# Batch 0 prepared by halves: what must stand before the first token tile, and what moves into it

## The chip, the cores and the metric

The kernel runs on one core of a Trainium2 chip. The core has TensorE (PE), VectorE (DVE), ScalarE (ACT), GpSimd (POOL) and SyncE (SP); each runs its own instructions in order, and they wait for each other by semaphores. The metric is the device time of one execution in microseconds.

## The reference

Two attentions with softmax, then two feed-forward blocks, all in float32. B = 8 batches, H = 8 heads, 576 tokens of 64 dimensions a head, 32 packed queries `p`:

```
p_packed = softmax(p @ k^T / 8) @ v          # 32 x 64 a head
attn     = softmax(q @ p_packed^T / 8) @ p_packed
x        = attn as 4608 tokens x 512
xn       = x / sqrt(mean(x * x) + 1e-6) * rms_g
y        = (silu(xn @ w_gate) * (xn @ w_val)) @ w_out     # 512 -> 1536 -> 512
h        = y @ w_in                                        # 512 -> 2048
out      = (max(h, 0) + alpha * min(h, 0)) @ w_out2        # 2048 -> 512
```

## The kernel before

The first block runs over 16 token tiles of 288 tokens: `tile(b, half, at)`, two halves for each of 8 batches. The second block runs over 9 tiles of 512 tokens and is not touched. A product in the tiles is three matmuls: every operand is split into a rounded `hi` part and a rest `lo` (`three_passes`, L476 to L478: hi x hi, lo x hi, hi x lo).

The value projection of the second attention is folded into the weights: for each batch `folded` (L606) multiplies the packed values by `w_gate` and `w_val`; the result m (12 blocks of 256 columns for two groups of heads) is split into `m_hi` and `m_lo`. Six folds, `fold0` to `fold5`, give two blocks each. A tile then multiplies the normed probabilities `an_hi`, `an_lo` by m.

Before tile 0 batch 0 is prepared on all engines (I call it the preparation). In order: scores of `p` against the keys in two halves (L497), copy to SBUF (L759), maximum, exp, sum, division (L919 to L934), transposes (L510), packed values (L523), their transpose, token scores for both halves (L548), transposes back (L951), softmax over 32 keys in each half (`shift`, `probs`, `sums`, `turn_p`), attention output `x` (L575) only for its squares (L795), two sums on POOL (L418, L420), a mean by a matmul with a constant (L584), `rsqrt` as exp of -0.5 ln (L803, L805) and one Newton step on DVE, `normed` on POOL (L424), and the split into `an_hi` (ACT, L811) and `an_lo` (DVE, L1006). The first preparation is `beside(0, name)` for a list of names on each of PE, ACT and DVE; those lists are the order in their queues. POOL's order is written out below `const_in`; after batch 0's steps it splits the twelve `w_out` chunks (`ow_hi` L436, `ow_lo` L438). Batch c = 1 to 7 is prepared inside the two tiles of batch c - 1: `PE_PLACES`, `DVE_PLACES` and `ACT_PLACES` name the work for each place of a tile, as `(half, where, step)`.

A tile has 12 steps f: products of gate and value (12 matmuls), Silu on ACT, the product `act_sb` on DVE (L1052), `h_hi` (ACT, L859) and `h_lo` (DVE, L1055); two steps later 12 matmuls with `w_out` accumulate the output. In PE's stream the places are "within" (between gate and value), "after", and "between" (after the output's matmuls).

Before some steps of the preparation PE runs fillers (`keep_busy`, L691): fp32 matmuls of a constant, whose result nobody reads, two instructions each; six of them stand last before tile 0. All loads go through SP's queue in the order of the code: p, k in two pieces, v, q, two small tables, four pieces of w_gate and w_val (`gv`), then a wait for the token scores, two pieces of w_out (`ow`), and batch 1's p and k.

## Time and profile before

| | |
|---|---|
| median of 3 timed runs | 1590.81 us (1589.01 to 1592.89) |
| the profiled execution | 1593.56 us, its span 1591.8 us |
| PE busy | 1566.0 us, 98% of the span |
| DVE, ACT, POOL busy | 727.9, 487.7, 206.2 us |
| mean granted PE clock | 0.992 |
| DMA | 76.18 MB, 48 GB/s over the span |

### The profile page before, as it was taken

Reading aid. Unit: us, or ns where it says so; the run is one execution under the profiler, and the core shown is the slowest. Engines: PE = TensorE matmul, PEld = TensorE weight load, DVE = VectorE, ACT = ScalarE, POOL = GpSimd, SP = SyncE. Lnnn points to the kernel's source line nnn. Section 1 sums busy time; section 2 is a strip of 40 time slices with the busy share of each in tenths; the row PEclk is TensorE's granted clock in tenths of the full one; section 3 lists DMA queues with packets and bytes.
Section 4 is the critical chain, followed back from the end, with each engine's and each line's share of the span. In section 5 each row is a group of like instructions: output and inputs, shape, how many; then the busy total and the mean of one; then the engine's idle time right before and its main releaser. Section 6 shows DMA issues by size and latency. Waiting matters only on the chain.

```text
span 1591.8 us, 25845 instructions
## 1 busy us (share of the span) xinstructions
PE 1566.0 (98%) x10390; PEld 1319.4 (83%) x10390; DVE 727.9 (46%) x1264; ACT 487.7 (31%) x913; POOL 206.2 (13%) x148
## 2 busy tenths in 40 slices
PE   6999999999999999999999999999999999999998
PEld 2688979888898888979988888888888888888887
DVE  4555454554545555454453334344434434343343
ACT  3445445463545545443211111111111111111111
POOL 1701010010100001013670101010100101010000
PEclk8899999999999999999999999999999999999999
DMA  9111202121030211103130101010000001010000
GB/s 356 66 46 47 73 5 77 45 77 46 2 107 16 77 46 46 44 3 148 42 121 0 54 0 53 0 40 13 26 26 26 26 0 53 0 53 0 23 4 27
DMA packets 38627, 76.18 MB, mean 48 GB/s; under 512 B 2192, under 2 KB 11408, under 8 KB 38544
## 3 DMA queue, kind: packets, MB, share of 16 engines
q1 hardware_dynamic: 33360, 65.55, 11.9%
q10 hardware_dynamic: 5184, 9.44, 1.5%
q8 instruction: 62, 1.02, 0.3%
q14 instruction: 21, 0.17, 0.0%
HBM read 56.11 MB, written 18.87 MB: 47 GB/s over the span
## 4 chain that ended last, share of the span: by engine, by line
PE 94%; DVE 3%; ACT 1%; issue 1%; POOL 0%; ACTq 0%; DVEq 0%; POOLq 0%
PE psum L476 30%; PE psum L477 28%; PE psum L478 28%; PE psum L606 2%; PE psum L575 1%; PE psum L691 1%; PE psum L497 1%; DVE m_lo L1012 1%; PE psum L523 1%; PE psum L548 1%; PE psum L584 1%; PE psum L510 1%; DVE h_lo L1055 1%; DVE act_sb L1052 0%; ACT h_hi L859 0%
## 5 line engine op out<-in xcount | busy, mean ns | idle before, releaser
L1088 DVE TENSOR_TENSOR h_lo<-g,h_hi 128x512 fp32r<-128x512 f32 x144 | 124.5, 865 | 453.0 <-ACT h_hi L886 453.0
L886 ACT CAST h_hi<-g 128x512 fp32r<-128x512 f32 x144 | 89.4, 621 | 637.3 <-PE psum L478 570.7
L476 PE MATMUL psum<-an_hi,m_hi 128*128 128x288 f32 x768 | 236.7, 308 | 3.7 <-DVE act_sb L1052 3.7
L476 PE MATMUL psum<-h_hi,ow_hi 128*128 128x288 f32 x768 | 235.9, 307 | 0.0
L477 PE MATMUL psum<-h_hi,ow_lo 128*128 128x288 f32 x768 | 227.2, 296 | 0.0
L477 PE MATMUL psum<-an_hi,m_lo 128*128 128x288 f32 x768 | 226.7, 295 | 0.0
L478 PE MATMUL psum<-h_lo,ow_hi 128*128 128x288 f32 x768 | 225.8, 294 | 0.0
L478 PE MATMUL psum<-an_lo,m_hi 128*128 128x288 f32 x768 | 225.7, 294 | 0.0
L1052 DVE TENSOR_TENSOR act_sb<-act_sb,psum 128x288 f32<-128x288 f32 x192 | 86.9, 453 | 190.2 <-PE psum L478 181.7
L476 PEld LDWEIGHTS psum<-an_hi,m_hi 128*128 128x128 f32 x768 | 144.0, 187 | 36.0 <-issue 28.5
L476 PEld LDWEIGHTS psum<-h_hi,ow_hi 128*128 128x128 f32 x768 | 144.1, 188 | 34.8 <-issue 33.5
L1055 DVE TENSOR_TENSOR h_lo<-act_sb,h_hi 128x288 fp32r<-128x288 f32 x192 | 104.7, 546 | 101.7 <-ACT h_hi L859 101.2
L477 PEld LDWEIGHTS psum<-h_hi,ow_lo 128*128 128x128 f32 x768 | 144.6, 188 | 0.4
L477 PEld LDWEIGHTS psum<-an_hi,m_lo 128*128 128x128 f32 x768 | 144.4, 188 | 0.6 <-issue 0.2
L478 PEld LDWEIGHTS psum<-h_lo,ow_hi 128*128 128x128 f32 x768 | 144.5, 188 | 0.0
L478 PEld LDWEIGHTS psum<-an_lo,m_hi 128*128 128x128 f32 x768 | 144.3, 188 | 0.0
L476 PE MATMUL psum<-xs,w_hi_front 128*128 (+1 forms) x360 | 140.1, 389 | 0.5 <-ACT y_sb L869 0.5
L476 PE MATMUL psum<-h_hi,w_hi_front 128*128 128x512 f32 x360 | 140.6, 391 | 0.0
L478 PE MATMUL psum<-h_lo,w_hi_front 128*128 128x512 f32 x360 | 140.1, 389 | 0.0
L477 PE MATMUL psum<-h_hi,w_lo_front 128*128 128x512 f32 x360 | 140.1, 389 | 0.0
L477 PE MATMUL psum<-xs,w_lo_front 128*128 (+1 forms) x360 | 140.0, 389 | 0.0
L478 PE MATMUL psum<-xs,w_hi_front 128*128 (+1 forms) x360 | 140.0, 389 | 0.0
(124 smaller groups left out, 2427.2 us busy)
## 6 DMA issues: line engine op xcount, KB each, us to landing
k_sb<-k_t SPq DMA_DIRECT2D x16, 576.0 KB, 4.6
q_sb<-q_t SPq DMA_DIRECT2D x8, 1152.0 KB, 6.4
y_mid<-y_sb SPq DMA_DIRECT2D x16, 576.0 KB, 3.4
xs_raw<-y_mid SPq DMA_DIRECT2D x9, 1024.0 KB, 5.2
out_t<-o_sb ACTq DMA_DIRECT2D x36, 256.0 KB, 2.0
v_sb<-v_s SPq DMA_DIRECT2D x8, 1024.0 KB, 6.5
gv_sb<-w_gv SPq DMA_DIRECT2D x4, 1536.0 KB, 18.2
w_raw_front<-w SPq DMA_DIRECT2D x2, 2560.0 KB, 13.0
```

The costliest lines, as they stand in the source:

```text
L476: nc.tensor.matmul(dst, w_hi, hi, start=start, stop=False)
L477: nc.tensor.matmul(dst, w_lo, hi, start=False, stop=False)
L478: return nc.tensor.matmul(dst, w_hi, lo, start=False, stop=stop)
L497: mm = nc.tensor.matmul(scores_ps[PACK * pair:PACK * (pair + 1), e, :], p_sb[dims, pair, :], k_sb[dims, pair, h * HALF:(h + 1) * HALF], st ...
L510: mm = nc.tensor.transpose(at_ps[t][:, at:at + P], a_sb[:, g, KEY_STARTS[j]:KEY_STARTS[j] + P], ident[:])
L523: mm = nc.tensor.matmul(pp_ps[PACK * pair:PACK * (pair + 1), e * HEAD_DIM:(e + 1) * HEAD_DIM], a_t[:, j, col:col + PACK], v_sb[:, j, head ...
L548: mm = nc.tensor.matmul(s2_ps(e)[PACK * pair:PACK * (pair + 1), :], pp_t[dims, pair, :], q[dims, pair, h * HALF:(h + 1) * HALF], start=Tru ...
L606: mm = nc.tensor.matmul(psum[keys, m_bank(c, j) + e, :].rearrange("p (f n) -> p f n", f=2), pp_tg[dims, pair, :], gv_sb[dims, 2 * j:2 * j ...
L886: nc.scalar.copy(h2_hi[:, f % 2, :], g32[:, f % 2, :]).then_inc(g_hi_done, 1)
L1052: nc.vector.tensor_tensor(act_sb[:, s, :], act_sb[:, s, :], val_ps, ALU.mult).then_inc(h32_done, 1)
L1055: nc.vector.tensor_tensor(h_lo[:, s, :], act_sb[:, s, :], h_hi[:, s, :].bitcast(F32), ALU.subtract).then_inc(h_lo_done, 1)
L1088: nc.vector.tensor_tensor(h2_lo[:, s, :], g32[:, s, :], h2_hi[:, s, :].bitcast(F32), ALU.subtract).then_inc(g_lo_done, 1)
```

## The change

Batch 0's preparation before tile 0 keeps half 0's chain, and the six folds. Half 1's `sums`, `probs`, `turn_p`, x2, x3, mean, rsqrt, Newton, norm and split get places in tile 0 (`PE_FIRST`, `DVE_FIRST`, `ACT_FIRST`), with the second halves of fold2 on DVE and of fold5's copy on ACT. Folds 3 to 5 are copied whole by ACT into `m_raw`, and POOL splits them (`split_m`), between the chunks of `w_out`. For batch 0 scores stay in PSUM (the maximum and exp read them there), the two POOL sums become a mean of four accumulating matmuls, half 0 is normed by DVE (`normed0`), half 1's `shift` subtraction is POOL's. k is loaded by halves of keys, `ow` in three pieces without a wait. Six fillers before the tile go, others come between. The diff, cut to what the prediction speaks of:

```diff
-FILLERS = {"scores0": 3, "scores1": 1, "turn_a01": 2, "packed": 1, "turn_packed": 1, "tokens0": 1, "tile": 6}
+PE_FIRST = {
+    (0, "after", 3): ["x2"], (0, "between", 3): ["x3"], (0, "between", 4): ["mean1"],
+}
+DVE_FIRST = {
+    (0, "within", 0): ["fold2"], (0, "after", 1): ["sums1"], (0, "between", 1): ["probs1"], (0, "after", 2): ["turn_p1"],
+    (0, "within", 5): ["mean1"], (0, "between", 7): ["newton1", "normed1"], (0, "within", 10): ["split1"],
+}
+ACT_FIRST = {
+    (0, "after", 0): ["fold5"], (0, "after", 3): ["x2"], (0, "between", 3): ["x3"],
+    (0, "between", 6): ["rsqrt1"], (0, "within", 9): ["split1"],
+}
+EARLY_BANK, LATE_BANK = 7, 0
+FILLERS = {"scores0": (3, EARLY_BANK), "scores1": (1, EARLY_BANK), "turn_a01": (4, EARLY_BANK),
+           "packed": (1, LATE_BANK), "turn_packed": (1, LATE_BANK), "tokens0": (1, LATE_BANK),
+           "x0": (2, LATE_BANK), "fold2": (1, LATE_BANK), "fold3": (1, LATE_BANK), "fold5": (1, LATE_BANK)}
+SPLIT_BY_POOL = 3
...
+        m_raw = place("m_raw", [P, NF1, GROUPS, GV], F32, at=m_lo_at)
...
-        q0_sb = place("q0_sb", [P, PAIRS, SEQ], at=ow_at)
+        q0_at = ow_at + 4 * 3 * MODEL
+        q0_sb = place("q0_sb", [P, PAIRS, SEQ], at=q0_at)
+        rinv_0 = place("rinv_0", [P, 2, HALF], at=q0_at + 4 * PAIRS * SEQ)
+        mean_0 = place("mean_0", [P, 2, HALF], at=q0_at + 4 * PAIRS * SEQ + 2 * step)
+        e2_0 = place("e2_0", [P, 2, GROUPS, HALF], at=q0_at + 4 * PAIRS * SEQ + 4 * step)
...
+        sq_0 = place("sq_0", [P, PAIRS, HALF], at=y_at)
...
+            return 0 if first(c) and i == 0 else 2
         def m_bank(c, j):
...
-            return 4 + 2 * (j % 2) if first(c) else 2
+            return [4, 6, 4, 6, 2, 6][j] if first(c) else 2
+
...
                 def at(where, f):
+                    if c == 1:
+                        for name in starting.get((half, where, f), []):
+                            beside(0, name)
...
-                for g in range(GROUPS):
-                    pairs = slice(2 * g, 2 * g + 2)
-                    sp.dma_start(k_sb[:, pairs, :],
-                                 k_t[b].rearrange("(c p) s -> p c s", p=P)[:, pairs, :]).then_inc(k_in[g], 16)
+                for h in range(2):
+                    keys = slice(h * HALF, (h + 1) * HALF)
+                    sp.dma_start(k_sb[:, :, keys],
+                                 k_t[b].rearrange("(c p) s -> p c s", p=P)[:, :, keys]).then_inc(k_in[h], 16)
...
-            sp.dma_start(g_sb[:], rms_g).then_inc(const_in, 16)
-            sp.dma_start(alpha_sb[:], alpha).then_inc(const_in, 16)
+            sp.dma_start(g_sb[:], rms_g).then_inc(g_in, 16)
...
-            sp.wait_ge(s2_mm, 2)
-            for n in range(2):
-                chunks = slice(n * NF1 // 2, (n + 1) * NF1 // 2)
+            for n in range(3):
+                chunks = slice(n * NF1 // 3, (n + 1) * NF1 // 3)
                 sp.dma_start(ow_raw[:, chunks, :], w1_o[chunks].rearrange("f p n -> p f n")).then_inc(ow_in[n], 16)
+            sp.dma_start(alpha_sb[:], alpha).then_inc(alpha_in, 16)
+            sp.wait_ge(scores_mm, 2)
...
+            def shift1():
+
+                pool.wait_ge(sub2_done, 1)
+                pool.wait_ge(s2_turned, 4)
+                pool.wait_ge(max2_done, 2)
+                rows = e2_0[:, 1].rearrange("p g s -> p (g s)").rearrange("p (b k) -> p b k", k=PACK)
+                nc.gpsimd.tensor_tensor(rows, rows, max2[:, 1, :].unsqueeze(2).to_broadcast([P, GROUPS * BLOCKS, PACK]),
+                                        ALU.subtract).then_inc(sub2_done, 1)
+
+            def split_m(j):
+
+                n = j - SPLIT_BY_POOL
+                blocks = slice(2 * j, 2 * j + 2)
+                pool.wait_ge(m_raw_done, n + 1)
+                nc.gpsimd.tensor_copy(m_hi[:, blocks], m_raw[:, blocks]).then_inc(m_part, 1)
+                pool.wait_ge(m_part, n + 1)
+                nc.gpsimd.tensor_tensor(m_lo[:, blocks], m_raw[:, blocks], m_hi[:, blocks].bitcast(F32),
+                                        ALU.subtract).then_inc(m_split, 1)
+
+            pool.wait_ge(g_in, 16)
             scaled(0)
-            squares(0, 0)
-            normed(0, 0)
-            squares(0, 1)
-            normed(0, 1)
+            shift1()
+            split_m(3)
             for f in range(NF1):
-
-                pool.wait_ge(ow_in[f // (NF1 // 2)], 16)
+                if f == 3:
+                    split_m(4)
+                    pool.wait_ge(s2_mm, 2)
+                if f == 5:
+                    split_m(5)
+                if f == 7:
+                    pool.wait_ge(a2n_done, 2)
+                pool.wait_ge(ow_in[f // (NF1 // 3)], 16)
                 nc.gpsimd.tensor_copy(ow_hi[:, f, :], ow_raw[:, f, :]).then_inc(ow_hi_done, 1)
                 pool.wait_ge(ow_hi_done, f + 1)
                 nc.gpsimd.tensor_tensor(ow_lo[:, f, :], ow_raw[:, f, :], ow_hi[:, f, :].bitcast(F32),
...
+                pe.wait_ge(k_in[h], 16 * (c + 1))
                 if h == 0:
-                    for g in range(GROUPS):
-                        pe.wait_ge(k_in[g], 16 * (c + 1))
                     pe.wait_ge(p_in, 16 * (c + 1))
-
-                    reached(pe, mean_copied, 2 * c)
-                    reached(pe, m_lo_done, NF1 * c)
-                else:
-                    pe.wait_ge(scores_out, 2 * c + 1)
+                    if c == 1:
+
+                        pe.wait_ge(m_raw_done, 2)
+                    elif c > 1:
+                        pe.wait_ge(mean_copied, 2 * c)
...
-                        mm = nc.tensor.matmul(scores_ps[PACK * pair:PACK * (pair + 1), e, :], p_sb[dims, pair, :],
+                        dst = psum[PACK * pair:PACK * (pair + 1), 2 * e + h if first(c) else 2 + e, 0:HALF]
...
-                nc.tensor.matmul(mean_ps, mean_w[:], sq[:, 0, :], start=True, stop=True).then_inc(mean_mm, 1)
+                if first(c):
+                    for pair in range(PAIRS):
+                        pe.wait_ge(squared, 1 + pair // 2 if h == 0 else 4)
+                        mm = nc.tensor.matmul(mean_ps(c, h), mean_w[:], sq_0[:, pair, :], start=pair == 0,
+                                              stop=pair == PAIRS - 1)
+                    mm.then_inc(mean_mm, 1)
...
                 if first(c):
                     pe.wait_ge(gv_in[(2 * j + 1) * W1_GROUPS // NF1], 16)
-                    reached(pe, m_lo_done, 2 * (j - 1))
+                    if j in (2, 3):
+                        pe.wait_ge(m_lo_done, 2 * (j - 1))
+                    if j == 4:
+                        pe.wait_ge(squared, 2)
+                    if j == 5:
+                        pe.wait_ge(m_raw_done, 1)
...
-                        if half == 0:
-                            pe.wait_ge(m_lo_done, NF1 * b + 2 * (f // 2) + 2)
+                        if half == 0 and b == 0 and f // 2 >= SPLIT_BY_POOL:
+                            pe.wait_ge(m_split, f // 2 - SPLIT_BY_POOL + 1)
+                        elif half == 0:
...
+                        if n == 0 and d == 0:
+                            pe.wait_ge(m_lo_done, 2 * SPLIT_BY_POOL)
+                            pe.wait_ge(m_raw_done, SPLIT_BY_POOL)
...
-            def keep_busy(count):
+            def keep_busy(count, bank):
                 for _ in range(count):
-                    nc.tensor.matmul(psum[:, 1, :].rearrange("p (a n) -> p a n", n=P), mean_w[:],
+                    nc.tensor.matmul(psum[:, bank, :].rearrange("p (a n) -> p a n", n=P), mean_w[:],
                                      ident[:].unsqueeze(1).to_broadcast([P, BANK // P, P]), start=True, stop=True)
-            pe.wait_ge(consts_set, 4)
-            for name in ("scores0", "scores1", "turn_a01", "turn_a2", "packed", "turn_packed", "tokens0", "tokens1"):
-                keep_busy(FILLERS.get(name, 0))
-                if name in ("scores0", "scores1", "tokens0", "tokens1"):
+            pe.wait_ge(consts_set, 2)
+            for name in ("scores0", "scores1", "turn_a01", "turn_a2", "packed", "turn_packed", "tokens0", "fold0", "tokens1",
+                         "fold1", "x0", "x1", "mean0", "fold2", "fold3", "fold4", "fold5"):
+                if name in FILLERS:
+                    keep_busy(*FILLERS[name])
+                if name in ("scores0", "scores1", "tokens0", "tokens1") or name[:4] == "fold":
                     beside(0, name + "_ready")
                 beside(0, name)
-            for name in ("fold0", "fold1", "fold2", "x0", "x1", "fold3", "mean0", "x2", "x3", "fold4", "fold5", "mean1"):
-                if name[:4] == "fold":
-                    beside(0, name + "_ready")
-                beside(0, name)
-            keep_busy(FILLERS["tile"])
             tiles_of_a(pe, tile, beside)
...
                 act.wait_ge(m_mm, NF1 // 2 * c + j + 1)
+                if first(c) and j >= SPLIT_BY_POOL:
+                    bank = m_bank(c, j)
+                    nc.scalar.copy(m_raw[:, 2 * j:2 * j + 2].rearrange("p f e n -> p e f n"),
+                                   psum[:, bank:bank + 2, :].rearrange("p e (f n) -> p e f n", f=2)).then_inc(m_raw_done, 1)
+                    return
...
-            for name in ("scores0", "scores1", "exp0", "exp1", "turn_a0", "turn_a2", "packed", "probs0", "fold0", "probs1",
-                         "fold1", "fold2", "x0", "x1", "fold3", "rsqrt0", "x2", "x3", "split0", "fold4", "fold5", "rsqrt1"):
+            for name in ("exp0", "exp1", "turn_a0", "turn_a2", "packed", "probs0", "fold0", "fold1", "x0", "x1", "probs1",
+                         "rsqrt0", "fold2", "fold3", "silu", "split0", "fold4"):
...
-                dve.wait_ge(scores_out, 2 * c + 2)
-                nc.vector.tensor_reduce(negmax[:, g:g + 1], a_sb[:, g, :], AXIS.X, ALU.max,
-                                        negate=True).then_inc(max1_done, 1)
+                if first(c):
+                    dve.wait_ge(scores_mm, 2)
+                    nc.vector.tensor_reduce(negmax[:, g:g + 1], scores0_of(g), AXIS.XY, ALU.max,
+                                            negate=True).then_inc(max1_done, 1)
...
+            def normed0(h):
+                dve.wait_ge(newton_step, 3 * h + 3)
+                nc.vector.tensor_tensor(a2[:, h], a2[:, h], rinv_0[:, h, :].unsqueeze(1).to_broadcast([P, GROUPS, HALF]),
+                                        ALU.mult).then_inc(a2n_done, 1)
...
-            def folded(c, j):
-                for e in range(2):
-                    dve.wait_ge(m_hi_done, NF1 * c + 2 * j + e + 1)
+            def folded(c, j, parts=(0, 1)):
...
             for name in ("max0", "max1", "norm0", "norm1", "turn_a1", "packed", "turn_s0", "shift0", "turn_s1", "sums0",
-                         "probs0", "turn_p0", "shift1", "fold0", "sums1", "probs1", "turn_p1", "fold1", "fold2",
-                         "fold3", "mean0", "newton0", "split0", "fold4", "fold5", "mean1", "newton1"):
+                         "probs0", "turn_p0", "shift1", "fold0", "fold1e0", "mean0", "fold1e1", "newton0", "normed0",
+                         "split0"):
```

## Rows read from the trace of the kernel before

**Rows 1.** The page: busy time by engine (share of the span), instructions.
```profile
PE 1566.0 (98%) x10390; PEld 1319.4 (83%) x10390; DVE 727.9 (46%) x1264; ACT 487.7 (31%) x913; POOL 206.2 (13%) x148
```

**Rows 2.** Windows by stage: length, then busy time (instructions) of PE, PEld, DVE, ACT, POOL; clock, DMA share, GB/s.
```profile
7.36:24.86 17.50, 13.45 (x200) 5.57 (x199) 7.58 (x19) 5.09 (x11) 0.40 (x1) 1.00 1.04 380
24.86:27.84 2.98, 0.01 (x2) 0.00 (x0) 2.84 (x6) 0.78 (x2) 0.00 (x0) 1.00 1.03 412
27.84:46.69 18.85, 12.95 (x101) 3.46 (x101) 13.52 (x24) 12.00 (x20) 6.17 (x5) 0.50 0.86 316
46.69:51.73 5.04, 5.04 (x7) 2.03 (x6) 2.31 (x5) 2.31 (x4) 1.53 (x2) 0.50 0.00 0
```

**Rows 3.** Timeline of PE, 0 to 56 us: start, length, engine, line, what, count.
```profile
2.47 5.26 PE L691 MATMUL psum<-ident,mean_w 128*128 128x512 f32 x6 [2.47 <-POOL v_sb L397]
...
7.90 0.72 PE L497 MATMUL psum<-k_sb,p_sb 64*32 64x288 f32 x16 [0.17 <-issue]
...
10.26 1.98 PE L691 MATMUL psum<-ident,mean_w 128*128 128x512 f32 x4
...
16.20 0.44 PE L510 MATMUL psum<-ident,a_sb 128*128 128x128 f32 x2 [0.24 <-ACT a_t L773]
...
22.94 1.93 PE L606 MATMUL psum<-gv_sb,pp_tg 64*32 64x512 f32 x32
...
46.69 7.83 PE L691 MATMUL psum<-ident,mean_w 128*128 128x512 f32 x12
53.96 0.69 PE L476 MATMUL psum<-an_hi,m_hi 128*128 128x288 f32 x1
```

**Rows 4.** Timeline of DVE, 0 to 75 us.
```profile
11.18 0.75 DVE L919 TENSOR_REDUCE negmax<-a_sb 128x1 f32<-128x576 f32 x1 [11.18 <-ACT a_sb L759]
...
26.80 0.78 DVE L983 STREAM_TRANSPOSE a<-e 128x576 f32<-128x576 f32 x1
...
38.51 0.46 DVE L989 TENSOR_SCALAR mean_sb<-psum 128x288 f32<-128x288 f32 x1 [0.26 <-PE psum L584]
...
43.61 1.25 DVE L1006 TENSOR_TENSOR an_lo<-a,an_hi 128x576 fp32r<-128x576 f32 x1 [2.22 <-ACT an_hi L811]
...
57.88 0.46 DVE L1052 TENSOR_TENSOR act_sb<-act_sb,psum 128x288 f32<-128x288 f32 x1 [0.23 <-PE psum L478]
...
64.11 0.75 DVE L1006 TENSOR_TENSOR an_lo<-a,an_hi 128x576 fp32r<-128x576 f32 x1
...
71.39 1.29 DVE L1055 TENSOR_TENSOR h_lo<-act_sb,h_hi 128x288 fp32r<-128x288 f32 x1 [0.50 <-ACT h_hi L859]
```

**Rows 5.** Timeline of ACT, 33 to 44 us.
```profile
33.54 1.19 ACT L795 ACTIVATE sq<-psum 128x576 f32<-128x576 f32 x2
...
37.44 1.28 ACT L800 ACT_TABLE_LOAD   x1
...
42.91 0.67 ACT L811 CAST an_hi<-a 128x576 fp32r<-128x576 f32 x1 [1.92 <-POOL a L424]
```

**Rows 6.** Timeline of POOL, 36 to 75 us.
```profile
36.30 0.79 POOL L420 TENSOR_TENSOR sq<-sq 128x288 f32<-128x288 f32 x1
41.47 1.41 POOL L424 TENSOR_TENSOR a<-a,rinv 128x576 f32<-128x576 f32 x1 [4.38 <-DVE rinv L1001]
...
71.07 1.29 POOL L438 TENSOR_TENSOR ow_lo<-ow_raw,ow_hi 128x512 fp32r<-128x512 f32 x1
...
73.22 1.29 POOL L438 TENSOR_TENSOR ow_lo<-ow_raw,ow_hi 128x512 fp32r<-128x512 f32 x1
```

**Rows 7.** Timeline of PE's weight loads, 20.7 to 25 us.
```profile
23.67 0.29 PEld L606 LDWEIGHTS psum<-gv_sb,pp_tg 64*32 64x32 f32 x16 [0.57 <-DMA gv_sb<-w_gv]
```

**Rows 8.** Timeline of PE in tile 0 and the next, 70 to 126 us.
```profile
70.94 0.40 PE L476 MATMUL psum<-an_hi,m_hi 128*128 128x288 f32 x1 [0.91 <-DVE act_sb L1052]
...
117.21 0.71 PE L575 MATMUL psum<-a,pp 32*64 32x288 f32 x8
...
125.55 0.65 PE L584 MATMUL psum<-sq,mean_w 128*128 128x288 f32 x2
```

More of the change, by code:

```diff
@@ L212, in first, with e2_of, sq_of, mean_of @@
             return isinstance(c, int) and c == 0
+        def e2_of(c):
+            return e2_0 if first(c) else e2
+        def sq_of(c):
+            return sq_0 if first(c) else sq
+        def mean_of(c):
+            return mean_0 if first(c) else mean_sb
+        def rinv_of(c):
+            return rinv_0 if first(c) else rinv
+        def at_ps(c, t):
+            if t == 2:
+                return psum[:, 4 if first(c) else 2, 0:GROUPS * P]
+            return psum[:, 2 + t, :]
+        def mean_ps(c, h):
+            return psum[:, 1 if first(c) and h == 0 else 3, 0:HALF]
         def x_bank(c, i):
-            return 2 * (i % 2) if first(c) else 2
+            return 0 if first(c) and i == 0 else 2
         def m_bank(c, j):
-            return 4 + 2 * (j % 2) if first(c) else 2
+            return [4, 6, 4, 6, 2, 6][j] if first(c) else 2
+        def scores0_of(g):
+            return psum[:, 2 * g:2 * g + 2, 0:HALF]
+        def evicted(c):
+            return NF1 * c - 2 * SPLIT_BY_POOL if c else 0
         def y_ps(m):
@@ L579, in mean @@
             def mean(c, h):
-                if not first(c):
-                    pe.wait_ge(m_lo_done, NF1 * c + 6 + 4 * h)
-                pe.wait_ge(sq_part, 4 * c + 2 * h + 2)
-                nc.tensor.matmul(mean_ps, mean_w[:], sq[:, 0, :], start=True, stop=True).then_inc(mean_mm, 1)
+                if first(c):
[4 more added lines that the diff above has]
+                    mm.then_inc(mean_mm, 1)
+                else:
+                    pe.wait_ge(m_lo_done, evicted(c) + 6 + 4 * h)
+                    pe.wait_ge(sq_part, 4 * (c - 1) + 2 * h + 2)
+                    nc.tensor.matmul(mean_ps(c, h), mean_w[:], sq[:, 0, :], start=True, stop=True).then_inc(mean_mm, 1)
             def fold_ready(c, j):
@@ L763, in scores_exp @@
                 act.wait_ge(bias1_done, GROUPS * c + g + 1)
-                nc.scalar.activation(a_sb[:, g, :], a_sb[:, g, :], ACT.Exp, bias=bias1[:, g:g + 1],
-                                     scale=SCALE, accum_out=sum1[:, g:g + 1]).then_inc(exp1_done, 1)
+                nc.scalar.activation(halves(a_sb[:, g, :]), scores0_of(g) if first(c) else halves(a_sb[:, g, :]), ACT.Exp,
+                                     bias=bias1[:, g:g + 1], scale=SCALE,
+                                     accum_out=sum1[:, g:g + 1]).then_inc(exp1_done, 1)
             def turn_a(c, t):
-                if t == 0:
-                    reached(act, mean_mm, 2 * c)
+                if t == 0 and c > 1:
+                    act.wait_ge(mean_mm, 2 * c)
                 act.wait_ge(at_mm, 3 * c + t + 1)
@@ L772, in turn_a @@
                 dst = a_t[rows, 2 * t:min(2 * t + 2, CHUNKS), :]
-                nc.scalar.copy(dst.rearrange("p j n -> p (j n)"), at_ps[t][rows, :]).then_inc(at_act, 1)
+                nc.scalar.copy(dst.rearrange("p j n -> p (j n)"), at_ps(c, t)[rows, :]).then_inc(at_act, 1)
             def packed(c):
@@ L860, in tile @@
                     at("between", f)
-                    if half == 0 and f == 1:
+                    if half == 0 and f == 1 and b > 0:
                         split(b, 1)
@@ L1057, in tile @@
                     at("between", f)
-                    if half == 0 and f == 2:
+                    if half == 0 and f == 2 and b > 0:
                         split(b, 1)
```

109 lines of the change are left out of this document (66 added, 43 removed).

## Prediction, made before the changed kernel was run

> **What bounds the kernel now.** I read the page's list of engines first: PE is busy for 98% of the span [rows 1], so after the start the time is PE's own work, and only two things can move it: when the first token tile begins, and what PE does or waits for once it has begun. Then the windows by stage [rows 2]: up to 24.86 us PE runs mostly at full clock, then it stands still for 3 us and the granted clock goes to 0.50 (1.2 GHz of 2.4), where it stays through the rest of the preparation. The PE timeline [rows 3] shows how that ends: six fillers (12 instructions) from 46.69 us, in which the clock returns at 51.73, and the first matmul of the tile at 53.96. The DVE, ACT and POOL timelines [rows 4 to 6] give the chain in front of it: scores, softmax over keys, packed values, token scores, softmax, mean of squares, rsqrt and Newton, `normed`, `split0`. Of that only half 0 and `fold0` to `fold2` are needed by the first products; half 1 and folds 3 to 5 stand in the same queues.
>
> **The change, part by part.** I follow the new order of each engine with the durations of the rows; all times are from the start of the span.
>
> *Up to the keys' softmax.* PE now waits for two constants, not four: fillers start about 0.9 us earlier (1.55 instead of 2.47) and their six instructions of 5.26 us at 1.2 GHz end at 6.8 [rows 3]. `scores0` needs only the first half of the keys; the last k load of before was what `scores0` waited for at 7.90 (PE idle 0.17 there). `scores0` ends at about 8.0, one filler (1.98 for two, so 0.99) at 9.0, `scores1` at 9.7. The maximum is read straight from PSUM, so the copy is gone: it starts at 9.8 instead of 11.18 [rows 4], 1.35 earlier. Four fillers (4.0 us) end at 13.7, level with the normed scores. The last transposes no longer wait for ACT's copy (0.24 [rows 3]), so all that follows to the end of `turn_p0` is 1.6 earlier: 26.80 + 0.78 becomes 26.0 [rows 4]. Reading PSUM instead of SBUF could cost 0.1 or save 0.1 an operation; I take nothing.
>
> *Loads.* Splitting k by keys halves the pieces. I take 0.3 us later for all that lands behind it, bounds 0 and 0.6. The weight load for `fold1` lands when PEld waited for it, at 23.67 [rows 7], so about 23.9 now; two more gv loads of 1536 KB follow at about 400 GB/s [rows 2], so the last lands at 31.6, ahead of fold4. The ow loads are issued right behind and no longer wait for the token scores; the DMA engines are full until past 40 us either way (share 1.03, then 0.86 of 18.85 us, which is to 44 [rows 2]), so they land as before.
>
> *PE from there.* tokens0, fold0 (0.97, half of the 1.93 for two [rows 3]), tokens1 are done at 21.6; PE stands 2.3 us for gv; fold1 23.9 to 24.9; two fillers to 26.8; x0 and x1, about 0.5 each, to 27.8. Each Square is 0.6 [rows 5]. `mean0` is now four matmuls on PE instead of two POOL sums (1.41 + 0.79 [rows 6]) and one matmul: 4 x 0.56 (0.65 for one with its tail at full clock [rows 8]), done at 30.2. Bounds 1.9 and 2.6. Then filler, fold2, filler, fold3: 3.9, ending at 34.0.
>
> *Half 0's chain.* `mean_sb` starts at 30.3; before, `normed` started 2.96 after it (38.51 to 41.47 [rows 4, 6]); now it runs on DVE, in 0.76 instead of POOL's 1.41, done at 34.0. But `split0` has fold3's raw copy and a table load ahead of it on ACT: the copy, 1024 elements a partition, I put at 1.05 by the Square of 576 (0.6), bounds 0.9 and 1.3. So 34.1, copy to 35.15, table load 1.28 [rows 5] to 36.45, cast 0.67 to 37.15. The table load is put ahead of the tile so that Silu finds it loaded; it costs the chain 1.28.
>
> *The subtraction that ends it.* `an_lo` takes 0.75 on DVE when undisturbed, but 1.25 beside a POOL operation at 43.61 [rows 4]. In the tile an `h_lo` that starts at 71.39 ends at 72.68, 0.32 after the POOL subtraction of 71.07 + 1.29 [rows 4, 6]: the DVE operation with two SBUF inputs is held until POOL's is done. Now `split_m(3)` starts on POOL at 35.2, at the same moment as ACT's table load, and its operations are 1024 wide: cast about 1.2, subtraction 1.41 + 448 x 0.62/288 (the slope from 0.79 for 288 to 1.41 for 576 [rows 6]) = 2.4, that is from 36.4 to 38.8. `an_lo`, ready at 37.2, then ends at 39.1, not 37.95. The first tile matmul comes at 39.2, when fold4, filler and fold5 (34.0 to 36.9) are long done. That is 14.8 us before 53.96.
>
> The Trainium skill ("SBUF — State Buffer", section "Who interferes with whom") calls the shared port an exclusive lock for the whole instruction, for DVE operations with two SBUF inputs against POOL operations that read SBUF. The sum by the longest extra in the rows (0.83, on `h_lo`) would put the tile at 38.8; by the rule, with wider POOL operations, it is the 39.2 used. The rows at 71 us agree with the rule.
>
> *What the tile gets.* On PE: x2, x3 (0.71 each with tail [rows 8], 0.5 in a row) and `mean1` (2.3): 3.3 us added, all of it on the path, since PE is the bound. On ACT and DVE: fold2's halves, fold5's copy, two Squares, a table load pair, `sums1`, `probs1`, `turn_p1`, Newton, `normed1`. ACT and DVE have time in a step of 3.2 us, but in step 2 `probs1` and an `h_lo` stand in DVE's queue ahead of the product that PE's step 3 needs; before, the product of step 1 ended 4.4 after the tile's first matmul (57.88 + 0.46 [rows 4]), now at 43.6; `sums1` 1.3, `h_lo` 0.46, `probs1` 0.76 and the product 0.46 bring it to 46.6, and PE asks at about 48.2. So undisturbed it is 1.6 in time; behind one cast and subtraction of `split_m(4)` (3.6, less 0.5 that they overlap) it is 1.5 late. I take 0.7, between the two. The stall of 0.91 at step 5 [rows 8] goes: `mean1` fills PE there. Key loads for batch 1 fall due at 43 us, when they land; I take nothing, bound 0.5. POOL's 12 units of cast and subtraction repeat every 2.15 (71.07 to 73.22 [rows 6]); with three double ones among them they end near 73 at that price, and unit n is always 2 us or more ahead of PE. Unit 7 waits for `normed1`; by my order it is ready about 1.7 before PE's step 9 asks.
>
> *Sum.* 14.8 earlier, minus 3.3, minus 0.7, plus 0.9: 11.7 us. The profiled execution took 1593.56 us (span 1591.8, 1.8 around it), so it becomes 1581.9; it lay 2.75 above the median of the timed runs, 1590.81, so I predict 1579.1. Everything behind tile 0 has the same instructions and keeps its time.
>
> **Rivals.** (1) *The clock falls in the preparation.* For it: in the rows it fell after PE had stood idle for 3 us behind light work [rows 2]; the new order has a 2.3 us gap for gv between small matmuls, and another just ahead of the tile. Against it: in 7.36 to 24.86 it stayed up with PE busy 13.45 of 17.5 and gaps in it. Price: fold1, two fillers, x and mean0 at half speed put 5 us on the chain (a filler is 1.75 instead of 0.99, a mean of 0.56 double that), and the folds some more unless the clock returns first: 5.5 in all, 1584.6. The Trainium skill ("TensorE: Matmul & The Clock Gate", section "HAM oscillation — how this bites in real kernels") says that waits between groups of matmuls bring the gate back down; that speaks for this rival, and the trace's fall at 27.84 agrees.
> (2) *Nothing is held by POOL.* If the operations miss each other, the tile starts at 38.0 and step 3 does not stall: 1.2 + 0.7 more, 1577.2.
> (3) *DVE's queue in tile 0 becomes the bound.* If the 1.5 of step 3 comes back in each of the eight steps up to the last one with added work, 11 us are given back: 1590, no change. Against it: the heavy steps are few.
> (4) *POOL becomes the bound, slower than before.* It has 18 units (three double ones count two each) between 35.2 and PE's last step of tile 0 near 81. At 2.15 they end at 74. Above 2.55 a unit PE starts to wait; above 3.2 the wait exceeds the 11.7 gained. With DVE's new two-input operations in the same steps holding POOL in turn, 3.6 a unit gives 18 x 3.6 + 35 = 100, 19 late: 1598. The longest pair in the rows is far from that.
>
> **Chances.** Forecast 0.60 (its own range 1576 to 1582), rival 1 0.19, rival 2 0.12, rival 3 0.05, rival 4 0.04. The range 1575.0 to 1585.0 holds the first three with their costs' bounds (mean 0.4, loads 0.3, copy 0.3, stall 0.7) and leaves out the last two. A measurement of this kernel tells about 0.2%, 3.2 us, from no change. Faster by more than that 0.91, within 0.05, slower 0.04.
>
> **What would show it.** In the profile after: scores' maximum near 9.8 us; PEld waiting for gv near 23.9; `mean_sb` at 30.3 and no POOL sum before it; an `an_lo` longer than 1 us that ends right behind a POOL subtraction of 2.4 us; first tile matmul at 39.2 with the granted clock at 1.00 throughout from 8 us on; one idle of PE around 48 us behind `act_sb`; nothing different from tile 1 on. A clock of 0.50 anywhere between 24 and 45 us means rival 1; idle of PE behind `ow_lo` or `m_lo` of POOL means rival 4; a first tile matmul later than 45 us makes the prediction wrong.

## The result, and the profile after

The kernel after took 1587.70 us, median of 12 runs (1586.31 to 1588.86), beside 1590.70 for the kernel before on the same chip (12 runs, 1588.82 to 1593.05): a ratio of 0.9982 (0.9973 to 0.9990). It is faster by 3.0 us, not by 11.7, and lies above the range of 1575 to 1585. Its profiled execution took 1586.99 us (span 1585.2), 6.6 less than the profiled one of before.

The page's list of engines, after, answers to [rows 1]: PE has almost the same work in a shorter span.

```profile
PE 1566.3 (99%) x10404; PEld 1321.6 (83%) x10404; DVE 734.6 (46%) x1259; ACT 487.4 (31%) x909; POOL 211.5 (13%) x149
```

The windows by stage of the kernel after (columns as in [rows 2]):

```profile
7.03:23.02 15.99, 13.61 (x188) 5.91 (x186) 7.90 (x19) 4.05 (x10) 0.40 (x1) 1.00 1.04 385
23.02:25.03 2.01, 2.01 (x17) 0.68 (x18) 1.87 (x5) 1.25 (x3) 0.00 (x0) 0.72 1.03 410
25.03:27.30 2.27, 2.27 (x4) 0.67 (x2) 2.27 (x5) 0.30 (x1) 1.06 (x1) 0.50 1.02 410
27.30:40.57 13.27, 10.14 (x95) 3.50 (x94) 5.93 (x9) 8.88 (x12) 4.15 (x4) 1.00 1.06 376
40.57:44.37 3.80, 3.80 (x17) 3.80 (x18) 1.60 (x3) 1.58 (x3) 3.64 (x5) 0.55 0.83 278
```

The reader is to see two falls of the granted clock to 0.50 (1.2 GHz): one in the preparation, one as the tile begins. Both come within 1 us after PE had stood idle for 2 us or more, which its timeline after shows (start, length, what, count, idle before; answers to [rows 3]):

```profile
23.02 1.18 PE L704 MATMUL psum<-gv_sb,pp_tg 64*32 64x512 f32 x16 [2.01 <-DMA gv_sb<-w_gv]
24.13 3.54 PE L794 MATMUL psum<-ident,mean_w 128*128 128x512 f32 x4
27.61 0.74 PE L662 MATMUL psum<-a,pp 32*64 32x288 f32 x16
29.09 2.21 PE L671 MATMUL psum<-sq,mean_w 128*128 128x288 f32 x8 [0.74 <-ACT sq L896]
...
40.57 0.40 PE L556 MATMUL psum<-an_hi,m_hi 128*128 128x288 f32 x1 [2.39 <-DVE an_lo L1126]
...
42.34 0.44 PE L558 MATMUL psum<-an_lo,m_hi 128*128 128x288 f32 x1
42.58 0.44 PE L556 MATMUL psum<-an_hi,m_hi 128*128 128x288 f32 x1
```

After 2.01 us without work (for gv, as in [rows 7]) two fillers take 3.54 where two took 1.98 [rows 3]. After 2.39 us for `an_lo`, the tile's matmuls come every 0.24 us. At 46 us they come every 0.13.

DVE after, 38 to 52 us (answers to [rows 4]), then ACT, 35 to 38 us, and POOL, 36 to 50 us (answer to [rows 5, 6]):

```profile
38.39 2.13 DVE L1126 TENSOR_TENSOR an_lo<-a,an_hi 128x576 fp32r<-128x576 f32 x1 [3.37 <-ACT an_hi L912]
...
47.50 2.53 DVE L1177 TENSOR_TENSOR h_lo<-act_sb,h_hi 128x288 fp32r<-128x288 f32 x1
49.95 1.16 DVE L1092 TENSOR_TENSOR e<-e,rcp 128x576 f32<-128x576 f32 x1
51.04 0.44 DVE L1174 TENSOR_TENSOR act_sb<-act_sb,psum 128x288 f32<-128x288 f32 x1
```

```profile
35.36 1.01 ACT L918 COPY m_raw<-psum 128x1024 f32<-128x1024 f32 x1 [1.00 <-PE psum L704]
36.39 1.28 ACT L949 ACT_TABLE_LOAD   x1
37.68 0.67 ACT L912 CAST an_hi<-a 128x576 fp32r<-128x576 f32 x1
```

```profile
36.43 1.04 POOL L498 CAST m_hi<-m_raw 128x1024 fp32r<-128x1024 f32 x1 [9.04 <-ACT m_raw L918]
37.55 2.35 POOL L500 TENSOR_TENSOR m_lo<-m_raw,m_hi 128x1024 fp32r<-128x1024 f32 x1
...
47.33 2.38 POOL L500 TENSOR_TENSOR m_lo<-m_raw,m_hi 128x1024 fp32r<-128x1024 f32 x1
```

`an_lo` (0.75 undisturbed) stands beside POOL's subtraction and takes 2.13. At 47.50 `h_lo`, 288 wide, takes 2.53 beside the next one; the product behind it is late at 51.04. PE's waits from 40 to 94 us, after (line, for what, us in total, times, longest), where [rows 8] had one of 0.91:

```profile
PE psum L556 <- DVE an_lo L1126: 2.4, 1, 2.4
PE psum L556 <- DVE h_lo L1177: 1.0, 1, 1.0
PE psum L594 <- DVE mean L1103: 0.4, 1, 0.4
PE psum L556 <- DVE act_sb L1174: 0.3, 1, 0.3
PE psum L556 <- DVE e L1063: 0.2, 1, 0.2
```

The product that is late at 51.04 is the 0.3 for `act_sb`. The 1.0 for `h_lo` is another one, in the tile's last step. These rows of POOL, DVE, ACT and PE are its chain: POOL takes up its last `w_out` chunks only at 76.22, behind `normed1`; beside one of them DVE's subtraction for batch 1 takes 1.40 (0.76 undisturbed, last fence); ACT's exp waits for it, and the cast `h_hi` stands behind the exp.

```profile
76.22 0.61 POOL L516 CAST ow_hi<-ow_raw 128x512 fp32r<-128x512 f32 x1 [13.93 <-DVE a L1121]
...
85.99 1.30 POOL L518 TENSOR_TENSOR ow_lo<-ow_raw,ow_hi 128x512 fp32r<-128x512 f32 x1
```

```profile
86.50 1.40 DVE L1078 TENSOR_TENSOR e<-e,max 128x576 f32<-128x576 f32 x1
```

```profile
87.99 1.28 ACT L884 ACT_TABLE_LOAD   x1 [1.09 <-DVE e L1078]
...
90.35 0.41 ACT L965 CAST h_hi<-act_sb 128x288 fp32r<-128x288 f32 x1
```

```profile
91.40 0.37 PE L556 MATMUL psum<-h_hi,ow_hi 128*128 128x288 f32 x1 [0.96 <-DVE h_lo L1177]
```

Before, with POOL idle from 84 to 99 us, the same subtraction of DVE:

```profile
93.53 0.76 DVE L964 TENSOR_TENSOR e<-e,max 128x576 f32<-128x576 f32 x1
```

I measure tile 0 from its first matmul to the issue of the store of its result, 0.69 us on the SP queue: before from 53.96 to 100.98, after from 40.57 to 93.83.

So the tile starts 13.4 earlier and takes 53.3 instead of 47.0.

### The profile page after: what moved, and what is told of

Same layout as the page of the kernel before. It is cut to its first block, busy times and chain, and to the rows that moved or that the text cites. A ratio compares the mean times of both kernels' runs of the same rounds, so it can differ in the third digit from the quotient of the medians.

```text
span 1585.2 us, 25879 instructions
## 1 busy us (share of the span) xinstructions
PE 1566.3 (99%) x10404; PEld 1321.6 (83%) x10404; DVE 734.6 (46%) x1259; ACT 487.4 (31%) x909; POOL 211.5 (13%) x149
## 4 chain that ended last, share of the span: by engine, by line
PE 92%; DVE 4%; ACT 1%; issue 1%; DMA 1%; SPq 0%; ACTq 0%; DVEq 0%
PE psum L556 29%; PE psum L557 28%; PE psum L558 28%; PE psum L704 2%; PE psum L662 1%; DMA gv_sb<-w_gv 1%; DVE h_lo L1177 1%; DVE act_sb L1174 1%; ACT h_hi L965 1%; DVE m_lo L1132 1%; PE psum L594 0%; PE psum L580 0%; PE psum L634 0%; PE psum L609 0%; PE psum L677 0%
## 5 line engine op out<-in xcount | busy, mean ns | idle before, releaser
L1210 DVE TENSOR_TENSOR h_lo<-g,h_hi 128x512 fp32r<-128x512 f32 x144 | 129.0, 896 | 448.6 <-ACT h_hi L992 448.6
```

The costliest lines, as they stand in the source:

```text
L1210: nc.vector.tensor_tensor(h2_lo[:, s, :], g32[:, s, :], h2_hi[:, s, :].bitcast(F32), ALU.subtract).then_inc(g_lo_done, 1)
```

## The experiments

Three questions came out of this. Is the kernel before's profiled execution a fair base? What do the two falls of the clock cost? What does POOL's subtraction cost? Every kernel has its ratio to before with its 95% interval. Each difference that is smaller than an interval is called so. The twelve kernels ran in three groups of four, and the kernel before, measured beside each, had medians of 1591.24, 1590.50 and 1591.31 us (1590.70 beside the kernel after). A difference of medians across groups is uncertain by up to 0.8 us more; the ratios are not.

**The kernel before, again.** No edit.

> The kernel before, unchanged, to see its runs one by one with span and mean granted clock. The profiles put the changed kernel 6.6 us ahead (1593.56 to 1586.99), the medians 3.0. Theory phase: the profiled run of before was a slow sample; its time scatters by 4 us because the stretch at 1.2 GHz in the preparation begins and ends at another point in each run. Then the slower runs have the lower mean clock, and in a new profile the first tile matmul (53.96 before) moves by 2 us or more with the length of the slow stretch (23.9 us before). Theory rest: the clock is the same in all runs and the 3.6 us come from elsewhere (after tile 0, or outside the span); then the first tile matmul stays within 0.5 us of 53.96 in a profile of any time.

Measured: 1590.77 us (1589.28 to 1593.37), ratio 0.9997 (0.9989 to 1.0006); the profiled execution took 1590.77. The windows of its preparation (clock third from the end):

```profile
14.00:17.70 3.70, 3.06 (x11) 2.39 (x12) 1.24 (x3) 0.95 (x2) 0.00 (x0) 0.54 1.03 407
27.88:34.71 6.83, 3.15 (x32) 0.58 (x32) 6.66 (x12) 3.08 (x6) 0.00 (x0) 0.50 1.04 389
38.12:44.95 6.83, 6.41 (x50) 1.47 (x50) 2.56 (x6) 3.87 (x8) 2.78 (x2) 0.50 0.83 297
```

Here the clock fell three times and came back in between; in [rows 2] it stayed at 0.50 from 27.84 to 51.73. The tile starts at 51.58, not 53.96. The same program falls at other moments in other executions, and its time follows: mean granted clock 0.995 goes with 1588.5 to 1589.3, 0.994 with 1588.8 to 1590.9, 0.993 with 1591.0 to 1592.8, 0.992 with 1592.8 to 1593.5. The prediction's base, 0.992 and 1593.56, was at the slow end of that.

**The kernel before without its six fillers.** `"tile": 6` becomes `"tile": 0`.

> The kernel before without the six fillers ahead of tile 0 (7.8 us of PE in its profile, 46.69 to 54.5). Theory clock: their place is taken by the tile's first products at 1.2 GHz, so little is won: the tile starts at about 47 instead of 52 to 54, runs its first 3.4 to 6.8 us at half speed (1.7 to 3.4 us lost), 1 to 3.5 us off the time. Rival: the fillers are pure cost, 5 to 7 us off, and then most of what the changed kernel gains (3.0) could be had by taking them out.

Measured: 1588.53 us (11 runs), ratio 0.9985 (0.9976 to 0.9994). Tile 0 starts at 45.17, 6.4 earlier than in the run above, and at full clock (1.00 from 45.17 to 50.50). But ACT is busy with half 1's rsqrt and then with Silu's table load until 49.09, and PE waits for the first Silu:

```profile
49.66 0.37 PE L476 MATMUL psum<-an_hi,m_hi 128*128 128x288 f32 x1 [2.53 <-ACT act_sb L853]
```

After that wait the granted clock is 0.51 from 50.50 to 54.00. The store is issued at 96.28 instead of 98.03. Leaving out the six alone gives 2.0 us; by the ratios this kernel and the kernel after (0.9982) are not told apart.

**The old order, with fillers to keep its clock up.** The six are left out and these come in:

```diff
+                if name == "fold2":
+                    keep_busy(5)
+                if name == "mean0":
+                    pe.wait_ge(squared, 1)
+                    keep_busy(1)
+                if name == "mean1":
+                    pe.wait_ge(squared, 3)
+                    keep_busy(2)
```

> The kernel before with its order kept, but fillers where PE stands idle (five ahead of fold2, one ahead of mean0, two ahead of mean1) and none of the six ahead of the tile. Nothing moves into tile 0. Theory clock: the preparation stays at 2.4 GHz, the chain to mean1 loses about 3 us and the tile starts at 43 to 44 at full speed, with none of the 3 us of x2, x3 and mean1 in the tile: 7 to 9 us off the time of before, more than the change's 3.0. Rival order: what counts is that half 1's chain stood ahead of the tile; then the clock alone gives under 3 us.

Measured: 1588.90 us (12 runs), ratio 0.9993 (0.9985 to 1.0002), tile from 46.52, where 7 to 9 us were expected. The fillers were too few in places: the clock still fell three times, for 10 us in all, the last time as the tile began. No gain over the run before. So whether the old order at full clock would reach the new one isn't shown; all that follows builds on the new order.

**Two fillers in the gap ahead of fold1.**

```diff
-           "x0": (2, LATE_BANK),
+           "fold1": (2, LATE_BANK), "x0": (2, LATE_BANK),
```

> The changed kernel with two fillers ahead of fold1, where PE stood 2.0 us for the gv load and the clock fell at 23.94 for 3.4 us. Theory clock: the clock stays up, x0 comes 0.8 earlier, mean 0.8 to 1.0 earlier, and the tile 0.8 to 1.3 earlier; the runs scatter less. Rival: fold1 is only moved by the fillers, which end at 23.0 + 0.3, nothing gained (0 to 0.3 slower).

Measured: 1584.60 us, ratio 0.9959 (0.9946 to 0.9972), 3.1 less than the kernel after. PE's timeline of this kernel:

```profile
23.26 1.09 PE L704 MATMUL psum<-gv_sb,pp_tg 64*32 64x512 f32 x16 [1.07 <-DMA gv_sb<-w_gv]
24.28 1.98 PE L794 MATMUL psum<-ident,mean_w 128*128 128x512 f32 x4
26.20 0.74 PE L662 MATMUL psum<-a,pp 32*64 32x288 f32 x16
```

With 1.07 us of idle time instead of 2.01 the clock stays up here in the preparation, x0 is 1.4 earlier, and the tile starts at 39.16: the 39.2 of the prediction. At the tile it falls as before, from 39.48 to 42.89.

**And two more ahead of the tile.** The line above and `keep_busy(2, LATE_BANK)` before `tiles_of_a`.

> The changed kernel with two fillers ahead of fold1 and two more ahead of tile 0, in the idle stretch of 2.4 us behind fold5; POOL's order is untouched, so an_lo is still held. It separates the clock from the lock. Theory two causes: against the kernel with fillers ahead of fold1 alone (1584.6) only the clock's fall at the tile goes, 3.4 us at half speed, so 1.6 to 1.8 off: 1582.9; the rest to 1580.0, 2.9, is the hold of an_lo and what follows it. Rival clock alone: 1580 to 1581, the hold costs nothing once the clock stays up.

Measured: 1583.79 us, ratio 0.9954 (0.9941 to 0.9968). The clock is at 1.00 all through the start, yet this is only 0.8 less than with the first pair (1.6 to 1.8 were expected), within the intervals, and in the profiles the store is no earlier (92.51 and 92.42). PE's waits in this kernel's tile 0 say why:

```profile
PE psum L594 <- DVE mean L1104: 1.1, 1, 1.1
PE psum L556 <- DVE act_sb L1175: 1.1, 1, 1.1
PE psum L556 <- DVE h_lo L1178: 0.9, 1, 0.9
PE psum L556 <- DVE an_lo L1127: 0.5, 1, 0.5
PE psum L556 <- DVE e L1064: 0.2, 1, 0.2
```

Within the tile 3.3 us are waited for, where it was 1.9. A faster PE meets DVE's queue, which POOL holds. For step 3's product (`act_sb`) it is now the product of `probs1` (0.76 undisturbed) that is held, by the second `split_m`:

```profile
46.13 2.97 DVE L1093 TENSOR_TENSOR e<-e,rcp 128x576 f32<-128x576 f32 x1
```

```profile
45.97 2.51 POOL L500 TENSOR_TENSOR m_lo<-m_raw,m_hi 128x1024 fp32r<-128x1024 f32 x1
```

**POOL's first `split_m` behind `an_lo`.**

```diff
             shift1()
+            pool.wait_ge(an_lo_done, 1)
             split_m(3)
```

> The changed kernel, but POOL begins split_m(3) only when an_lo of half 0 is done. In the profile after, an_lo (DVE) took 2.13 us and ended 0.6 behind POOL's 2.35 us subtraction. Theory lock: an_lo takes 0.75 us again, the first tile matmul comes at 39.2 instead of 40.57, 1.4 us earlier, and PE's idle ahead of it falls from 2.4 to 1.0 us, so that the clock may stay up as well: 1.3 to 3 us off the time. Rival: the 2.13 us are not POOL's doing, an_lo keeps them, no change. A second rival: POOL now runs 3.5 us later through tile 0 and PE waits for ow_lo or m_lo there: same time or slower.

Measured: 1584.33 us, ratio 0.9956 (0.9944 to 0.9968), 3.4 less than after. `an_lo` takes 0.76 and the tile starts at 39.33, though the clock still fell in the preparation (24.36 to 27.77). PE is idle for only 1.01 ahead of the tile, and the clock doesn't fall there.

**That, and the two fillers ahead of fold1.**

> The changed kernel with both single edits: split_m(3) waits for an_lo, and two fillers ahead of fold1. Each took 3.1 to 3.4 us off the changed kernel's median. Theory additive: first tile matmul at 38.0 in the profile (39.33 with one, 39.16 with the other, 40.57 with none), clock at full speed from 8 us on, and the median 1582.5 (5 us off the changed kernel), with runs within 1 us of each other. Rival: both act through the same event, the clock's fall ahead of the tile; then together they give 3.5 to 4 us, 1584.

Measured: 1580.02 us (1579.22 to 1580.98), ratio 0.9932 (0.9919 to 0.9945). That is 7.7 less than after (5 were expected), and in its profile the clock falls nowhere before the kernel's end. Its DVE, POOL and PE timelines around the tile's start:

```profile
36.56 0.76 DVE L1127 TENSOR_TENSOR an_lo<-a,an_hi 128x576 fp32r<-128x576 f32 x1 [3.37 <-ACT an_hi L913]
...
43.85 1.43 DVE L1178 TENSOR_TENSOR h_lo<-act_sb,h_hi 128x288 fp32r<-128x288 f32 x1
```

```profile
37.38 1.04 POOL L498 CAST m_hi<-m_raw 128x1024 fp32r<-128x1024 f32 x1 [10.06 <-DVE an_lo L1127]
...
43.69 1.28 POOL L519 TENSOR_TENSOR ow_lo<-ow_raw,ow_hi 128x512 fp32r<-128x512 f32 x1
...
47.47 1.27 POOL L498 CAST m_hi<-m_raw 128x1024 fp32r<-128x1024 f32 x1
```

```profile
37.37 0.40 PE L557 MATMUL psum<-an_hi,m_hi 128*128 128x288 f32 x1 [1.01 <-DVE an_lo L1127]
```

The start is 3.2 earlier than after's. The next `split_m`, now at 47.47, misses the `h_lo` that it held before; what holds that one is a subtraction of 1.28, and it takes 1.43.

**The Silu table load behind the cast.** In ACT's order `"silu", "split0"` becomes `"split0", "silu"`.

> The changed kernel, but on ACT Silu's table load stands behind split0's cast instead of ahead of it. The load takes 1.28 us on the chain to the first tile matmul, and the cast done 1.28 earlier lets an_lo start at about 37.1, before POOL's subtraction takes over at 37.55. Theory chain plus lock: first tile matmul at 38.0, 2.6 us earlier (1.28 for the load, 1.3 for the lock), and with PE idle for 1 us instead of 2.4 the clock stays up: 2.6 to 4.3 us off the time. Rival chain alone: 1.3 us off. Rival: the chain doesn't set the time, no change.

Measured: 1586.03 us (1583.02 to 1586.76), ratio 0.9966 (0.9954 to 0.9978). That is 1.7 less than after where 2.6 to 4.3 were expected, and the two intervals overlap. Its runs lie in two groups: 1583.0 and 1583.5 at clock 1.000, the others at 0.999 to 0.997. The profiled one (1583.02) starts its tile at 36.41, the earliest but one of all, and then PE waits 1.44 us for batch 1's keys, at 40.98. An earlier tile alone exposes that load. This profile has no filler ahead of fold1 and the longest gap for gv in any changed kernel, yet the clock stays at 1.00 behind it:

```profile
22.95 1.09 PE L704 MATMUL psum<-gv_sb,pp_tg 64*32 64x512 f32 x16 [3.02 <-DMA gv_sb<-w_gv]
```

So the length of a gap alone doesn't decide whether the clock falls.

**The keys ahead of `w_out`.** Batch 1's p and k, with the wait for batch 0's scores in front of them, are issued before the three `ow` loads. With the Silu load late and the fillers, without POOL's wait:

> The changed kernel with Silu's table load behind split0's cast, two fillers ahead of fold1, and batch 1's p and k loaded ahead of the three ow loads. With the table load late alone the tile started at 36.41 in the profile, but PE then stood 1.44 us for the k load of batch 1, and the runs scattered from 1583.0 to 1586.8. Theory loads: with k ahead of ow this wait goes, the clock stays up, and the median is 1581 to 1582, 6 us off the changed kernel. Rival: POOL then waits for ow or DVE's queue in tile 0 takes the gain back, 1583 or more.

Measured: 1582.10 us, ratio 0.9944 (0.9931 to 0.9957). The tile starts at 36.22, the wait for k is gone, but `mean` (1.2), `act_sb` (1.1) and `h_lo` (0.9) are waited for, as with both fillers above. With the keys first on top of the best kernel so far:

> split_m(3) behind an_lo, two fillers ahead of fold1 (together 1580.0), and batch 1's p and k loaded ahead of ow. In that kernel's profile PE waited 0.6 us in tile 0 for the k load of batch 1. Theory loads: 0.6 off, 1579.4. Rival: the wait for k only took the place of another behind it (act_sb of DVE), no change; or ow comes late to POOL and it gets slower, as the kernel with the early table load gone and k first (1582.1) might hint.

Measured: 1580.92 us, ratio 0.9933 (0.9920 to 0.9947): the 0.6 us wait for k goes, the time stays the same within the intervals. And with all four edits:

> As the one before, with Silu's table load behind split0's cast as well. It differs from the kernel at 1582.1 only in that POOL waits for an_lo before split_m(3). Theory: the tile starts at 36.1 in the profile, 1.3 earlier than the 37.4 of the 1580.0 kernel, and the time is 1578.3 (1.3 less than with k first alone). Rival DVE in tile 0: between tile start and step 5 DVE's queue with the moved work is the bound, so an earlier start turns into waits for act_sb and mean (0.4 to 1.2 us each were seen): 1580 to 1582.

Measured: 1579.46 us (1577.99 to 1580.17), ratio 0.9925 (0.9912 to 0.9939), the fastest of all, 11.9 us less than the kernel before measured beside it (1591.31). Its tile starts at 36.89 (36.1 was expected) and PE waits in it for `h_lo` (0.9) and `e` (0.2) alone. Against 1580.02 with two edits it isn't told apart.

**One matmul for half 1's mean.** The kernel with POOL late and the fillers at fold1, but the squares of three of the four pairs are left out of half 1's mean, to price what was moved onto PE.

```diff
-                    for pair in range(PAIRS):
+                    pairs = range(PAIRS) if h == 0 else range(1)
+                    for pair in pairs:
```

> split_m(3) behind an_lo and two fillers ahead of fold1 (together 1580.0), with one of the four matmuls of mean1 in tile 0; the squares of the other three pairs are left out of half 1's mean. It prices what was moved onto PE's path: in the profile the four take 2.10 us, one 0.65 with its tail. Theory path: 1.5 to 1.6 off, 1578.4. Rival: mean1 covers a wait for silu or act_sb that appears when it is shorter (0.9 at the same step before the change), so only 0.7 off, 1579.3.

Measured: 1582.11 us (1581.13 to 1584.28), ratio 0.9944 (0.9930 to 0.9957): 2.1 above the kernel with four matmuls for that half, though PE has three less and 1.5 us were to be gained. The intervals overlap, and the two kernels are of different groups, but all its five runs lie above the five of the other. In tile 0 the products behind `mean1` start 0.96 earlier (55.27 against 56.23), and the transposes behind them only 0.23 (57.81 against 58.04), with a wait of 0.35 for DVE's `mean` in between. Its store comes 0.2 earlier (88.51 against 88.72), and the time is lost 660 us later. DVE and PE of this kernel there, then the same of the kernel with four matmuls:

```profile
752.70 2.30 DVE L1179 TENSOR_TENSOR h_lo<-act_sb,h_hi 128x288 fp32r<-128x288 f32 x1 [0.50 <-ACT h_hi L967]
```

```profile
755.42 0.40 PE L557 MATMUL psum<-an_hi,m_hi 128*128 128x288 f32 x1 [1.30 <-DVE act_sb L1176]
```

```profile
753.02 1.32 DVE L1178 TENSOR_TENSOR h_lo<-act_sb,h_hi 128x288 fp32r<-128x288 f32 x1 [0.50 <-ACT h_hi L966]
```

```profile
754.76 0.40 PE L557 MATMUL psum<-an_hi,m_hi 128*128 128x288 f32 x1 [0.34 <-DVE act_sb L1175]
```

POOL splits the second weights there, its subtractions 2.4 us long. A shift of some tenths decides whether an `h_lo` meets one at its start or in its middle. That is 1.0 of the difference; the rest I can't assign.

## Why the prediction was wrong

**The base, 2.8 us: the step that failed first.** The prediction went from the profiled execution to the median by taking off the 2.75 that it lay above it. But those 2.75 were the long cold stretch of [rows 2], and the change removes that stretch. One can't take away the cold start as a gain and the excess that it caused once more. The two profiled executions of before differ by 2.8 us in all and by 2.95 at the store of tile 0, so the excess does lie before that point, 2.4 of it in the start. Before, as profiled again, lies on its median, and from there the same arithmetic gives 51.58 - 39.2 = 12.4 of start, not 14.8.

**The clock: rival 1 was right, twice, and its size wasn't.** The forecast had "the granted clock at 1.00 throughout". The 2.3 us gap for gv was foreseen and given 0.19. PE stood idle for 2.01 us and the clock fell, for 3.4 us. The tile start came at 40.57 instead of 39.2, and two fillers in that gap gave it back (39.16), so the other terms up to the tile hold: the mean of four matmuls (2.21 for eight instructions, 0.56 each), the raw copy (1.01 against 1.05), the table load, POOL's 1.04 and 2.35 (against 1.2 and 2.4). That it agrees to the tenth is partly luck: POOL's subtraction ended 0.3 earlier than forecast, and `an_lo` ended 0.6 after it, not 0.3. The rival's price was 5.5 on the start; the profiles show 1.4 there and the medians 3.1 for the whole run. The gap ahead of the tile was named in that rival too, but its price has nothing for a fall there; two fillers against it brought 0.8, within the intervals. The Trainium skill ("TensorE: Matmul & The Clock Gate", section "HAM oscillation — how this bites in real kernels") says that waits between groups of matmuls bring the gate down. Both gaps of over 2 us in the kernel after agree with that, but the gap of 3.02 with the Silu load late had no fall behind it.

**POOL's hold: right at `an_lo`; in the tile it was charged at step 3 alone.** I charged 1.2 at the start, 0.7 at step 3 and nothing for the other steps. Tile 0, from first matmul to store, was to take 47.0 + 3.3 + 0.7 - 0.9 = 50.1. By the same measure:

| kernel | start | store issued | tile 0 | median |
|---|---|---|---|---|
| before, profiled again | 51.58 | 98.03 | 46.5 | 1590.77 |
| after | 40.57 | 93.83 | 53.3 | 1587.70 |
| two fillers at fold1 | 39.16 | 92.42 | 53.3 | 1584.60 |
| both pairs | 39.04 | 92.51 | 53.5 | 1583.79 |
| POOL late, fillers at fold1 | 37.37 | 88.72 | 51.4 | 1580.02 |
| and Silu late, keys first | 36.89 | 87.46 | 50.6 | 1579.46 |

The 3.1 us over the forecast are the half-clock start (3.4 us at half speed, so 1.7 lost) and the waits, 1.9 us where 0.7 was charged; 0.2 is left over. The wait that was priced, step 3's, is 0.34 of the 1.9 (at full clock, with both pairs, 1.05). The others stand where the prediction put nothing, behind DVE operations that run beside POOL: `mean` (0.43, at 63.12) behind an `h_lo` of 1.29, `e` (0.19, at 79.34) behind an `h_lo` of 1.50, and `h_lo` (0.96, at 91.40) at the end of the chain from the 1.40 shown above. That last wait is in every changed kernel, at 0.91 to 0.96. I had put POOL's end near 73 us and had asked only whether PE would wait for its chunks, not what the last five, from 76 to 87 us, would hold. No kernel here was built to move those chunks, so the last wait's cause is read from rows and not shown by an experiment.

Taking away the half-clock start alone turns it into waits (both pairs). Only when POOL begins its splits later does the tile come to 51.4: the waits for `act_sb` (1.05) and `mean` (1.11) go, 0.59 for the keys comes, and 0.5 of the 2.1 stays unassigned. With the keys first and the Silu load late it is 50.6. Moving POOL gives 3.8 by the medians (1583.79 to 1580.02), 3.5 by the ratios; the kernel with POOL late doesn't have the fillers at the tile. In the profiles 1.7 of it is at the start of the tile and 2.1 in it. The Trainium skill ("SBUF — State Buffer", section "Who interferes with whom") has the lock for whole instructions: `h_lo` took 2.53 beside a POOL subtraction of 2.38. I used it for `an_lo` and for step 3, and not for DVE's operations in the other steps.

**In numbers.** The miss is 1587.7 - 1579.1 = 8.6: 2.8 the base, 1.4 the start, 3.1 tile 0, 0.6 behind it, and 0.7 because after's profiled execution lay below its median. The steps of the prediction that failed are thus the base (its excess taken off twice), the clock (put at 1.00 throughout), and the waits in tile 0 outside step 3 (put at nothing). In medians, fillers at fold1 (3.1), fillers at the tile (0.8) and POOL late in their place (3.8) lead from 1587.7 to 1580.0. Of the rivals, the second (nothing held) is out; the third (DVE's queue in tile 0) is right in kind, but in four waits that sum to 1.9 us, not eight of 1.5; the fourth didn't come. "Nothing different from tile 1 on" doesn't hold either: from the store to the end the span is 1490.8 us before, 1491.4 after, 1489.9 with POOL late and fillers, 1491.8 with one matmul for the mean. PE's waits for `act_sb` from 700 to 800 us, which go from 0.3 to 2.1 us over the kernels (1.2 before), are the part of this that a trace shows.

**What stays open.** Why two fillers move the medians by 3.1 and the store by 1.4: each kernel has one profile, and its other runs may fall at other moments. The 1.1 us that the one-matmul kernel loses beyond the shown 1.0. Whether the fillers ahead of the tile bring anything of their own. What, besides the length of a gap, decides whether the clock falls. Whether the old order with its clock kept up would have done as well.

## What to carry to other kernels

Before a gain read from one profiled execution is put on a median, look whether what sets that execution apart from the median is the very thing that the change removes; the mean granted clock of the runs tells it (here 0.992 to 0.995, and 5 us). Work that is moved to an engine with time to spare is to be priced by what it holds on the other engines, at every step where it runs. Here one line that starts a wide POOL subtraction later was worth 3.4 us, where the whole reorder had brought 3.0. When a start is pulled forward, look for the gaps of 2 us and more that it leaves in PE: two cheap matmuls in such a gap brought 3.1 us. Then look what the earlier tile waits for next; here it was the keys of the next batch, though loading them first brought nothing that the medians tell apart.
